# Moving bias, q and k loads, GpSimd's order and one weight split in a fused attention and two-MoE kernel

## The chip, the core and the metric

The kernel runs on one core of one Trainium2 chip. The metric is the device time of the whole launch in microseconds (us), lower is better. TensorE (PE) multiplies and transposes, VectorE (DVE), ScalarE (ACT) and GpSimd (POOL) work elementwise, and SyncE (SP) issues nearly all DMAs. Each engine runs its own instructions in order and waits on semaphores.

## What is computed

Attention with a learned relative bias, then two feed-forward layers. The reference, cut to what matters:

```python
# q, k, v: (4, 8, 576, 64); hidden = 32
scores = scale * np.matmul(q, k.transpose(0, 1, 3, 2))
rel = (pos[:, None] - pos[None, :])
x = (log1p(abs(rel)) / log1p(max(pos[:, None], 1)))[..., None]
bias = np.maximum(x @ w1 + b1, 0.0) @ w2          # (576, 576, 8)
scores = scores + bias.transpose(2, 0, 1)[None]
attn = softmax(scores)
o = attn @ v                                      # -> x: (2304, 512)
h = maximum(maximum(x @ m1, x @ m2), x @ m3)      # d_ff 768
x = h @ m_out
h = x @ m2_in                                     # d_ff 2048
g = where(h >= 1, h, where(h <= -1, 0, (h + 1)**2 / 4))
out = g @ m2_out
```

## The kernel before

Everything is float32. A product is made in three passes over a high part and a low part of each operand (`_hi` and `_lo`, rounded value and rest). The program has four stages: the bias, attention, the first feed-forward layer (C) and the second (D).

**Bias stage.** 36 steps `s` make 16 rows of the bias for all 8 heads each. Per step VectorE fills three quarters of the hidden tile (L830) and ScalarE one (`hidden_act`, L544), TensorE multiplies (L1027), ScalarE copies the result from PSUM into one of four staging buffers (`bias_copy`, L553), and SyncE stores it to `bias_scratch` in DRAM (`store_bias`, L362, 296 KB). The copy of step s may not start before the store of step s-4 has landed, which is the semaphore `bias_free[s % 4]`. The bias is then read back tile by tile: `first_bias(h, t, stored)` waits until the first `stored` stores have landed and loads tile t (128 rows, the last one 64) for head h of the pair, as one DMA (h = 0, L352, 288 KB) or two (h = 1, L354 and L355, 256 and 32 KB). All of this stands on SyncE's one queue in program order, between stores, together with `load_q` (four DMAs, L312 and L314) and `load_k` (five, L320 to L327) of the first pairs of heads.

**Attention.** 16 pairs of heads (`GROUPS`) with 5 row tiles each (`NT`) give 80 tiles. Work is laid out in slots `w` = 0 to 82: in slot w TensorE makes the scores of tile w (L941), turns the probabilities of tile w-3 (`turn_probs`, L954, and L968), turns q and k for a tile further on (`turn_rest`, L917) and does a piece of the product with v (L993). VectorE adds the bias and takes the row extreme (`add_bias`, L760), inverts the denominator of tile w-1 (L790), and copies half of the turned probabilities of tile w-3 (`copy_lower`, L774). ScalarE copies the other half (L589), copies turned q, k (`copy_turned`, L603 and L609) and takes the exponents (L577). GpSimd makes the high and low parts of turned q and k (`high_turned` L471, `low_turned` L480), normalises tile w-1 (`normalise`, L497), and prepares the denominator of tile w (`denominators`, L488). `high_turned(w)` waits, in every slot with w % 5 == 3, for the scores of tile w+1, since it overwrites what these read.

**Attention's end.** Weights of the layers come as units of 1024 columns: loaded into one of two buffers `raw`, split by ScalarE into the high part (`split_weights`, L639) and by VectorE (L823) or GpSimd (L516) into the low part. A load of unit u waits until unit u-2 is split. `W_SPLIT` is slot 75. Units 0 and 1 are split in slots 75 to 79; unit 2 only after the last output copy (L781) of attention, because its place in `w_all` overlaps attention tiles that are still in use. The slots 80 to 82 of TensorE already hold the first three products of layer C; the next ones (L1041) need unit 2.

## Time and profile before

| | us |
|---|---|
| median of 3 runs (1034.73 to 1037.45) | 1035.3 |
| the profiled execution | 1034.67 |
| its span | 1032.5 |
| TensorE busy in the span | 998.2 (97%) |
| VectorE / ScalarE / GpSimd busy | 506.6 / 493.5 / 294.8 |
| bias stage | 0 to 62 |
| attention | 62 to 329 |
| layers C and D | from 332 |

The profiled execution is 0.6 below the median and 2.2 above its own span. Since TensorE is busy nearly all the time from 77 us on, the columns to look at are the idle time before its instructions and what ended it; in the first 62 us TensorE, VectorE and ScalarE share the load, and the DMA engines are busy at 0.74 of the time.

### The profile page before, as it was taken

How to read it: one execution, taken by the hardware profiler on the slowest of the kernel's cores; microseconds unless marked ns; L12 is line 12 of the kernel's file. 1: busy time of each engine (PE TensorE's matmuls, PEld its weight loads, DVE VectorE, ACT ScalarE, POOL GpSimd, SP SyncE). 2: the span in 40 equal slices, each digit the busy share in tenths (PEclk: the TensorE clock that was granted, in tenths of full speed). 3: DMA queues.
4: the chain of work that ended last, by engine and by line, in shares of the span. 5: the costliest groups of instructions: out<-in, count | busy, mean ns of one | idle time of the engine just before them, and what ended most of it. 6: DMA issues, size and time to landing. Idle time of an engine off the chain costs nothing.

```text
span 1032.5 us, 20383 instructions
## 1 busy us (share of the span) xinstructions
PE 998.2 (97%) x7608; PEld 866.3 (84%) x7608; DVE 506.6 (49%) x1173; ACT 493.5 (48%) x1024; POOL 294.8 (29%) x506
## 2 busy tenths in 40 slices
PE   6779999999998999999999999999999999999998
PEld 4457666677666999999999999998989989899897
DVE  8867667666683231323131326754444444544543
ACT  7888777787793321212121325544343433433433
POOL 1048888888883720000000235700000000000000
PEclk9989999999999999999999999999999999999999
DMA  5872524425311410000000112300000000000000
GB/s 141 260 217 65 150 67 102 125 48 161 93 34 50 143 41 1 1 0 0 0 0 0 41 62 82 103 1 31 1 31 0 0 30 0 30 0 0 31 1 31
DMA packets 96042, 56.10 MB, mean 54 GB/s; under 512 B 64224, under 2 KB 81632, under 8 KB 95968
## 3 DMA queue, kind: packets, MB, share of 16 engines
q1 hardware_dynamic: 95872, 55.11, 19.0%
q8 instruction: 46, 0.75, 0.3%
q14 instruction: 28, 0.23, 0.1%
q10 hardware_dynamic: 96, 0.00, 0.0%
HBM read 39.46 MB, written 15.63 MB: 53 GB/s over the span
## 4 chain that ended last, share of the span: by engine, by line
PE 90%; DVE 5%; issue 2%; ACT 1%; POOL 1%; SPq 0%; DMA 0%; ACTq 0%; DVEq 0%
PE ps L1041 41%; PE ps L1100 19%; PE ps L1068 7%; PE ps L993 7%; PE ps L941 7%; PE ps L954 3%; DVE xT L830 2%; PE ps L1027 2%; PE ps L968 1%; DVE s_sb L760 1%; PE ps L917 1%; ACT probs L577 0%; POOL probs L497 0%; ACT xT L544 0%; DVE w_all L823 0%
## 5 line engine op out<-in xcount | busy, mean ns | idle before, releaser
L1041 PE MATMUL ps<-x_hi,w_all 128*128 128x384 f32 x1632 | 437.9, 336 | 3.0 <-DVE w_all L823 3.0
L1041 PEld LDWEIGHTS ps<-x_hi,w_all 128*128 128x128 f32 x1632 | 297.1, 188 | 8.9 <-issue 4.7
L1041 PE MATMUL ps<-x_lo,w_all 128*128 128x384 f32 x816 | 273.3, 335 | 0.0
L1100 PE MATMUL ps<-w_all,g_hi 128*128 128x512 f32 x576 | 179.8, 393 | 0.0
L1041 PEld LDWEIGHTS ps<-x_lo,w_all 128*128 128x128 f32 x816 | 153.2, 188 | 3.9
L516 POOL TENSOR_TENSOR w_all<-raw,w_all 128x256 fp32r<-128x256 f32 x100 | 77.6, 808 | 274.6 <-ACT w_all L639 274.6
L760 DVE CUSTOM_DVE_ANT_0 s_sb<-ps,bias_h 128x576 f32<-128x576 f32 (+1 forms) x160 | 114.5, 752 | 47.3 <-PE ps L941 40.4
L497 POOL TENSOR_SCALAR probs<-probs,row_inv 128x576 f32<-128x576 f32 (+1 forms) x160 | 121.9, 771 | 4.8 <-DVE row_inv L790 4.8
L1100 PEld LDWEIGHTS ps<-w_all,g_hi 128*128 128x128 f32 x576 | 106.4, 188 | 19.2 <-issue 1.2
L577 ACT ACTIVATE probs<-s_sb,row_min 128x576 f32<-128x576 f32 (+1 forms) x160 | 122.2, 769 | 0.0
L1100 PE MATMUL ps<-w_all,g_lo 128*128 128x512 f32 x288 | 113.9, 395 | 0.0
L701 ACT ACTIVATE ta<-ps 128x384 f32<-128x384 f32 x96 | 47.0, 490 | 115.5 <-PE ps L1041 114.9
L883 DVE TENSOR_SCALAR tb<-ta 128x384 f32<-128x384 f32 x96 | 38.0, 396 | 113.8 <-ACT ta L701 112.0
L891 DVE TENSOR_TENSOR g_lo<-tb,g_hi 128x384 fp32r<-128x384 f32 x96 | 56.6, 589 | 58.6 <-ACT g_hi L711 58.6
L850 DVE TENSOR_TENSOR tb<-ps,ta 128x384 f32<-128x384 f32 x36 | 20.0, 555 | 126.8 <-PE ps L1041 126.8
L711 ACT ACTIVATE g_hi<-tb 128x384 fp32r<-128x384 f32 x96 | 50.4, 524 | 63.8 <-DVE tb L889 63.8
L1068 PE MATMUL ps<-g_hi,w_all 128*128 128x384 f32 x288 | 78.8, 334 | 0.0
L993 PE MATMUL ps<-p_t,v_in 128*64 128x320 f32 (+1 forms) x512 | 76.0, 418 | 0.6 <-DVE xT L781 0.6
L589 ACT ACTIVATE p_t<-ps 128x512 f32<-128x512 f32 x80 | 47.7, 597 | 56.7 <-PE ps L954 55.2
L705 ACT ACTIVATE tb<-tb 128x384 f32<-128x384 f32 x96 | 50.4, 525 | 48.8 <-DVE tb L883 48.8
L677 ACT ACTIVATE g_hi<-tc 128x384 fp32r<-128x384 f32 x36 | 18.9, 524 | 112.5 <-DVE tc L857 112.5
L889 DVE TENSOR_TENSOR tb<-tb,tc 128x384 f32<-128x384 f32 x96 | 56.4, 588 | 32.2 <-ACT tb L705 31.8
(78 smaller groups left out, 1325.7 us busy)
## 6 DMA issues: line engine op xcount, KB each, us to landing
bias_scratch<-p_t SPq DMA_DIRECT2D x36, 296.0 KB, 3.8
raw<-in_moe_w_out SPq DMA_DIRECT2D x22, 256.0 KB, 3.0
bias_h<-bias_scratch SPq DMA_DIRECT2D x16, 288.0 KB, 4.2
raw<-in_moe_w SPq DMA_DIRECT2D x18, 256.0 KB, 3.1
out<-o_sb SPq DMA_DIRECT2D x18, 256.0 KB, 2.0
q_in<-in_q SPq DMA_DIRECT2D x32, 128.0 KB, 2.4
bias_h<-bias_scratch SPq DMA_DIRECT2D x16, 256.0 KB, 3.4
v_in<-in_v SPq DMA_DIRECT2D x32, 128.0 KB, 2.4
```

What stands on the lines that cost most here:

```text
L497: pool.tensor_scalar(pr, pr, row_inv[0:n, r, h:h + 1], 1.0, ALU.mult, ALU.mult).then_inc(p_norm, 1)
L516: last = pool.tensor_tensor(w_lo[:, at + c:at + c + PIECE], raw[:, u % 2, c:c + PIECE], w_hi[:, at + c:at + c + PIECE].bitcast(F32), ALU.s ...
L577: act.activation(probs[0:n, r, h * S:(h + 1) * S], s_sb[0:n, (2 * u + h) % 4, :], ACT.Exp, scale=-1.0, bias=row_min[0:n, r, h:h + 1], accu ...
L705: act.activation(tb[:, :], tb[:, :], ACT.Square, scale=0.5, bias=0.5).then_inc(d_sq, 1)
L760: dve.tensor_tensor_reduce(s_sb[0:n, (2 * u + h) % 4, :].rearrange("p (c x) -> p c x", c=2), ps[0:n, 2 * h:2 * h + 2, 0:HC], bias_h[0:n, h ...
L889: dve.tensor_tensor(tb[:, :], tb[:, :], tc[:, :], ALU.add).then_inc(d_g, 1)
L891: dve.tensor_tensor(g_lo[:, ft % 4, :], tb[:, :], g_hi[:, ft % 4, :].bitcast(F32), ALU.subtract).then_inc(d_g_ok, 1)
L941: ends = [pe.matmul(ps[:, 2 * h + c, 0:HC], a[HALVES[h], i % 2, 0, t * P:(t + 1) * P], b[HALVES[h], i % 2, 1, c * HC:(c + 1) * HC], start= ...
L993: last = pe.matmul(ps[h * HALF:(h + 1) * HALF, O_BANK_A, 0:cols.stop - cols.start], v_in[:, i % 2, h, kt, :], tqk[:, i % 2, 0, cols] if kt ...
L1041: last = pe.matmul(ps[:, bank, 0:BLK], w[:, at:at + P], x[:, kt, :], start=(kt == 0 and n == 0), stop=(kt == KT - 1 and n == 2))
L1068: last = pe.matmul(ps[:, Y_BANK + dt, 0:BLK], w[:, at:at + P], g[:, ft % 2, :], start=(opens and i == 0), stop=(closes and i == 2))
L1100: last = pe.matmul(ps[:, O_BANK + t, :], g[:, ft % 4, t * P:(t + 1) * P], w[:, wout_d(ft):wout_d(ft) + DM], start=(opens and i == 0), stop ...
```

## The change

There are five edits. In the diff the first `slot` is GpSimd's, the second ScalarE's. (1) SyncE loads tiles 1 (both heads) only after stores 33 and 34, and tiles 2 and 3 after the last store, instead of during the stage; tile 0 stays after stores 11 and 12. `load_v(0)` goes ahead of the tiles 4. (2) The q and k of the third pair, loaded after the stage before, are now loaded after store 22 (q) and store 26 (k). (3) In the first two slots ScalarE takes the exponents before it copies the turned q and k, and GpSimd normalises and prepares the denominator before it makes the high and low parts. (4) GpSimd has this second order also in every slot with w % 5 == 3. (5) `qk_hi` and `qk_lo` move behind the other tiles of attention in memory, so that unit 2's place is free after the last scores; its high part is made in slot 80 and its low part in slot 82, and unit 1's low part moves from slot 79 to slot 80.

```diff
             v_in = sb("v_in", [P, 2, 2, NT, D], c=att)
-            qk_hi = sb("qk_hi", [P, 2, 2, NT * P], F32R, c=att)
-            qk_lo = sb("qk_lo", [P, 2, 2, NT * P], F32R, c=att)
...
             row_inv = sb("row_inv", [P, RING, 2], c=att)
+            qk_hi = sb("qk_hi", [P, 2, 2, NT * P], F32R, c=att)
+            qk_lo = sb("qk_lo", [P, 2, 2, NT * P], F32R, c=att)
...
-                if i >= 2:
+                if i >= 3:
                     sp.wait_ge(lo_ok, NT * (i - 1))
...
-                if s > 4 and (s - 4) % 8 == 7:
-                    first_bias(0, (s - 4) // 8, s - 3)
-                if s > 4 and (s - 4) % 8 == 0:
-                    first_bias(1, (s - 4) // 8 - 1, s - 4)
-            first_bias(1, T - 1, NSUP - 4)
-            load_qk(2)
+                if s == 22:
+                    sp.wait_ge(lo_ok, NT)
+                    load_q(2)
+                if s == 26:
+                    load_k(2)
+                if s in (11, 12):
+                    first_bias(s - 11, 0, s - 3)
+                if s in (NSUP - 3, NSUP - 2):
+                    first_bias(s - NSUP + 3, 1, 2 * P // SUP)
+            for t in range(2, T):
+                for h in range(2):
+                    first_bias(h, t, (t + 1) * P // SUP)
+            sp.wait_ge(staged_zero, 1)
+            load_v(0)
             for h in range(2):
                 first_bias(h, T, NSUP)
-            sp.wait_ge(staged_zero, 1)
-            load_v(0)
...
             def slot(w):
-                high_turned(w)
-                if w < 2:
-                    low_turned(w)
+                late = w < 2 or w % NT == 3
+                if not late:
+                    high_turned(w)
                 if w:
                     normalise(w - 1)
                 if w < NU:
                     denominators(w)
-                if w >= 2:
-                    low_turned(w)
+                if late:
+                    high_turned(w)
+                low_turned(w)
...
             def slot(w):
-                copy_turned(w)
+                if w >= 2:
+                    copy_turned(w)
                 if w < NU:
                     exponent(w, 0)
                     exponent(w, 1)
+                if w < 2:
+                    copy_turned(w)
...
-                if w in (W_SPLIT, W_SPLIT + 2):
+                if w in (W_SPLIT, W_SPLIT + 2, W_SPLIT + 5):
                     split_weights((w - W_SPLIT) // 2)
             act.wait_ge(o_ok, PAIRS)
-            split_weights(2)
...
-                if w in (W_SPLIT + 2, W_SPLIT + 4):
-                    low_weights((w - W_SPLIT - 2) // 2)
+                if w - W_SPLIT in (2, 5, 7):
+                    low_weights((2, 5, 7).index(w - W_SPLIT))
             output(GROUPS - 1, 0)
             output(GROUPS - 1, 1)
-            low_weights(2)
```

SyncE's queue from the tenth to last store of the bias stage on, before (after the k load of the second pair; `x7` are stores 21 to 27, then 29 to 35):

```order
34 L362 DMA bias_scratch<-p_t 16x8x592 x7
35 L352 DMA bias_h<-bias_scratch 128x576
36 L362 DMA bias_scratch<-p_t 16x8x592
37 L354 DMA bias_h<-bias_scratch 128x512
38 L355 DMA bias_h<-bias_scratch 128x64
39 L362 DMA bias_scratch<-p_t 16x8x592 x7
40 L352 DMA bias_h<-bias_scratch 128x576
41 L354 DMA bias_h<-bias_scratch 128x512
42 L355 DMA bias_h<-bias_scratch 128x64
43 L312 DMA q_in<-in_q 128x4x64
```

The same place now (`x4` are stores 23 to 26, `x7` are 27 to 33; four q DMAs stand ahead of the first row):

```order
34 L362 DMA bias_scratch<-p_t 16x8x592 x4
35 L320 DMA k_in<-in_k 128x4x64
36 L322 DMA k_in<-in_k 64x64
37 L325 DMA k_in<-in_k 64x4x64
38 L326 DMA k_in<-in_k 64x4x64
39 L327 DMA k_in<-in_k 64x64
40 L362 DMA bias_scratch<-p_t 16x8x592 x7
41 L352 DMA bias_h<-bias_scratch 128x576
42 L362 DMA bias_scratch<-p_t 16x8x592
43 L354 DMA bias_h<-bias_scratch 128x512
44 L355 DMA bias_h<-bias_scratch 128x64
45 L362 DMA bias_scratch<-p_t 16x8x592
```

The k load now stands between store 26 and store 27, and no bias load stands between store 12 and store 33.

GpSimd in its fourth slot (w = 3), before: high part, two normalisations, denominator, low part:

```order
27 L471 TENSOR_SCALAR qk_hi<-tqk 128x2x128
28 L497 TENSOR_SCALAR probs<-probs,row_inv 128x576 x2
29 L488 TENSOR_SCALAR row_den<-row_sum 128x2
30 L480 TENSOR_TENSOR qk_lo<-tqk,qk_hi 128x2x128
31 L471 TENSOR_SCALAR qk_hi<-tqk 128x2x128
```

The same slot now (the functions stand six lines further down in the file):

```order
27 L503 TENSOR_SCALAR probs<-probs,row_inv 128x576 x2
28 L494 TENSOR_SCALAR row_den<-row_sum 128x2
29 L477 TENSOR_SCALAR qk_hi<-tqk 128x2x128
30 L486 TENSOR_TENSOR qk_lo<-tqk,qk_hi 128x2x128
31 L477 TENSOR_SCALAR qk_hi<-tqk 128x2x128
```

The high part, which waits for TensorE, moved behind the denominator. The same happens in slots 8, 13 and so on up to 68.

VectorE at attention's end (from slot 79's copy of turned probabilities), before; L823 is a low part of a weight unit, L781 an output copy:

```order
573 L774 COPY p_t<-ps 128x8x64 [waits py_ps]
574 L823 TENSOR_TENSOR w_all<-raw,w_all 128x1024 [waits w_ok,w_hi_ok]
575 L781 COPY xT<-ps 128x320 [waits o_ps]
576 L790 RECIPROCAL row_inv<-row_den 128x2 [waits p_norm,den_ok]
577 L774 COPY p_t<-ps 128x8x64 [waits py_ps] x2
578 L781 COPY xT<-ps 128x256 [waits o_ps]
579 L781 COPY xT<-ps 128x320 [waits o_ps]
580 L823 TENSOR_TENSOR w_all<-raw,w_all 128x1024 [waits w_ok,w_hi_ok]
```

And now (L832 is the low part, L790 the output copy, L783 the copy of turned probabilities, L799 the inverse):

```order
573 L783 COPY p_t<-ps 128x8x64 [waits py_ps]
574 L790 COPY xT<-ps 128x320 [waits o_ps]
575 L799 RECIPROCAL row_inv<-row_den 128x2 [waits p_norm,den_ok]
576 L783 COPY p_t<-ps 128x8x64 [waits py_ps]
577 L832 TENSOR_TENSOR w_all<-raw,w_all 128x1024 [waits w_ok,w_hi_ok]
578 L783 COPY p_t<-ps 128x8x64 [waits py_ps]
579 L832 TENSOR_TENSOR w_all<-raw,w_all 128x1024 [waits w_ok,w_hi_ok]
580 L790 COPY xT<-ps 128x256 [waits o_ps]
```

The output copy is no longer behind unit 1's low part, and unit 2's low part stands ahead of both last output copies instead of behind them.

## Rows read from the trace of the kernel before

**Rows 1.** Windows: us, then each engine's busy time, PE clock, DMA share, GB/s.
```profile
0.00:62.20 62.20, 46.62 (x894) 26.97 (x894) 49.65 (x116) 51.27 (x78) 3.43 (x16) 1.00 0.74 211
62.20:77.40 15.20, 11.09 (x106) 9.02 (x106) 8.82 (x26) 11.67 (x28) 11.00 (x22) 0.78 0.71 185
77.40:300.00 222.60, 217.06 (x2644) 154.38 (x2643) 157.19 (x440) 177.07 (x430) 189.56 (x352) 1.00 0.38 96
...
332.00:1032.50 700.50, 695.97 (x3708) 656.52 (x3706) 273.66 (x553) 236.43 (x451) 77.37 (x100) 1.00 0.08 25
```

**Rows 2.** Waits, 24 to 62.2 us: who waited for whom: total, times, longest.
```profile
ACT p_t L553 <- DMA bias_scratch<-p_t: 5.5, 5, 2.8
```

**Rows 3.** Timeline of ScalarE: start, us, ..., [idle before <- what ended it].
```profile
46.29 0.76 ACT L553 ACTIVATE p_t<-ps,nconst 128x592 f32<-128x592 f32 x1 [0.38 <-DMA bias_scratch<-p_t]
...
48.43 0.75 ACT L553 ACTIVATE p_t<-ps,nconst 128x592 f32<-128x592 f32 x1 [0.73 <-DMA bias_scratch<-p_t]
...
49.75 0.74 ACT L553 ACTIVATE p_t<-ps,nconst 128x592 f32<-128x592 f32 x1
...
56.99 0.75 ACT L553 ACTIVATE p_t<-ps,nconst 128x592 f32<-128x592 f32 x1 [0.42 <-DMA bias_scratch<-p_t]
```

**Rows 4.** Timeline of SyncE's queue around the second pair's k load.
```profile
31.75 0.60 SPq L320 DMA_DIRECT2D k_in<-in_k  x1
...
35.40 1.24 SPq L362 DMA_DIRECT2D bias_scratch<-p_t  x2
```

**Rows 5.** DMA issues, last us to landing: the stores issued at 24.9 and 35.4.
```profile
bias_scratch<-p_t SPq DMA_DIRECT2D x1, 296.0 KB, 3.1
...
bias_scratch<-p_t SPq DMA_DIRECT2D x1, 296.0 KB, 4.0
```

**Rows 6.** The same view: store 33 (issued at 60.7), tile 3's last piece (64.6).
```profile
bias_scratch<-p_t SPq DMA_DIRECT2D x1, 296.0 KB, 4.2
...
bias_h<-bias_scratch SPq DMA_DIRECT2D x1, 32.0 KB, 4.0
```

**Rows 7.** Timeline at attention's start: scores of tiles 3, 4; bias add of tile 3.
```profile
69.37 0.40 PE L941 MATMUL ps<-qk_hi 64*128 64x288 f32 x2 [1.55 <-DVE row_min L760]
...
71.90 0.75 DVE L760 CUSTOM_DVE_ANT_0 s_sb<-ps,bias_h 128x576 f32<-128x576 f32 x1
...
72.81 0.61 PE L941 MATMUL ps<-qk_hi 64*128 64x288 f32 x2
```

**Rows 8.** Timeline of GpSimd, VectorE, TensorE in a group in the middle.
```profile
153.86 0.40 POOL L471 TENSOR_SCALAR qk_hi<-tqk 128x256 fp32r<-128x256 f32 x1 [1.56 <-PE ps L941]
...
156.02 0.17 DVE L790 RECIPROCAL row_inv<-row_den 128x2 f32<-128x2 f32 x1 [0.86 <-POOL row_den L488]
156.10 0.67 DVE L774 COPY p_t<-ps 128x512 f32<-128x512 f32 x1
...
156.42 0.29 PE L941 MATMUL ps<-qk_lo,qk_hi 64*128 64x288 f32 x2
156.55 0.29 PE L941 MATMUL ps<-qk_hi,qk_lo 64*128 64x288 f32 x2
156.92 0.28 PE L954 MATMUL ps<-ident,probs 64*128 64x64 f32 x2
```

**Rows 9.** Waits, 84 to 300 us.
```profile
PEld ps L954 <- issue: 3.6, 13, 0.3
```

**Rows 10.** Timeline of attention's end.
```profile
312.84 1.21 DVE L823 TENSOR_TENSOR w_all<-raw,w_all 128x1024 fp32r<-128x1024 f32 x1
...
314.60 1.08 PE L993 MATMUL ps<-p_t,v_in 128*64 128x256 f32 x8 [0.56 <-DVE xT L781]
...
329.21 1.06 ACT L639 ACTIVATE w_all<-raw 128x1024 fp32r<-128x1024 f32 x1 [5.57 <-DVE xT L781]
330.18 0.47 ACT L666 ACTIVATE ta<-ps 128x384 f32<-128x384 f32 x1
...
331.63 0.41 PE L1041 MATMUL ps<-x_hi,w_all 128*128 128x384 f32 x1 [2.99 <-DVE w_all L823]
```

## The prediction

> **What bounds the kernel now.** I read the busy times by stretch first [rows 1]. From 332 us on TensorE is busy for 695.97 of 700.5 us, so nothing before it matters there except when it begins. From 77.4 to 300 it is busy for 217.06 of 222.6: about 5.5 us idle, which an order of the other engines can give back. The first 62.2 us are another thing: TensorE 46.6, VectorE 49.7, ScalarE 51.3, DMA share 0.74. There ScalarE's copies wait for stores, 5.5 us in 5 waits [rows 2]. The stretch from 62.2 to 77.4 is the ramp of attention: TensorE has 4.1 of 15.2 us idle and a mean granted clock of 0.78. The end of attention has one large gap, 2.99 us [rows 10]. The change touches all four places, and since TensorE sets the end from 77 us on, what each place gives to or takes from TensorE adds up.
>
> **Bias stage.** A copy of step s needs the store of step s-4. Of the 5.5 us, three waits of 0.38, 0.73 and 0.42 (1.5 us) come after 46 us [rows 3]. The other two (5.5 - 1.5 = 4.0, one of them 2.8) come earlier, from tile 0's loads and the second pair's k load, and both loads stay where they are: cost unchanged. The waits at 46.29 and 48.43 are those for stores 20 and 21, which shared the DMA engines with tile 1's loads. Those loads leave, so 0.38 + 0.73 = 1.1 us go, and copy 26 starts at 48.65 instead of 49.75 and ends at 49.4.
>
> What comes in their place is the k load after store 26. The five DMAs keep SyncE for 35.40 - 31.75 = 3.65 us [rows 4], so from 49.4 + 0.6 on it is occupied until about 53.3, and store 27 goes out only then. A store that follows such a load landed after 3.1 us (behind a q load) or after 4.0 (behind the k load) [rows 5]: store 27 lands at 56.4 to 57.7. Copy 31 needs it. Without any wait it would start at 56.99 - 0.42 - 1.1 = 55.5 [rows 3], so it waits for 0.9 to 2.2 us and starts at 56.4 to 57.7, against 56.99 before. From the copy of step 31 on ScalarE works through without a wait. The stage ends 0.6 us earlier to 0.7 later; I take **0.0**, the middle. The new q load after store 22 delays store 23 in the same way by some 2.4 us, but copy 27 falls at about 50 and store 23 should have landed at 50.1 to 51; I put this into the range (up to +1.0), not the sum.
>
> A rule speaks against this exchange. The q and k rows are 64 floats, 256 bytes, whereas a bias row has 2304. The trace shows no penalty of its own: the store behind four q DMAs took 3.1 us, as short as the shortest. The Trainium skill (DMA: Bandwidth & Descriptors, Why small descriptors are slow (HBM only)) gives a fixed per-packet cost that makes a 256-byte one about 27% dearer. By that rule the q and k loads would cost the engines an extra quarter of their bytes' time, which would make the stage's term the upper end instead of zero.
>
> **First tiles.** Tiles 1 to 3 now come after store 33. Store 33 went out at 60.7 and landed 4.2 later, at 64.9; tile 3's last piece went out at 64.6 and landed at 68.6 [rows 6]. Between the two landings lie two stores and two loads, 3.7 us, 0.93 each. Now two stores and six loads lie behind store 33: 8 x 0.93 = 7.4 us, tile 3's last piece lands at 72.3; with loads a little dearer than stores, at 73. The bias of tile 3 is added after it, 0.75 us a head [rows 7] (the scores of tile 3 started at 69.37 after waiting 1.55 us for tile 2's add), and the scores of tile 4 start after that, at 73.1 to 73.8, instead of 72.81. Tile 2's last piece lands two loads earlier, at 70.4 to 71, so tile 3's scores start at 71.2 to 71.8 instead of 69.37, and everything TensorE does behind them until tile 4 (3.4 us before) comes later by that, if it does not find time: 73.8 to 75.2. ScalarE's and GpSimd's new order takes a wait away here, since normalising tile 0 no longer stands behind the low parts of slot 1; it is hidden, because the loads are last. About half of the lag falls into the time at half clock, and counts half at full clock. I take **+1.0** (0 to +2.4).
>
> **GpSimd's fourth slot.** Before, GpSimd waits 1.56 us for the scores of tile w+1 with the normalisation and the denominator behind it. So VectorE's inverse waits 0.86 us for the denominator, the copy behind it ends at 156.10 + 0.67 = 156.77, and TensorE's transposes, which need that copy, issue at 156.92 [rows 8]. The two score instructions ahead of them stand 0.13 apart; the transposes follow after 0.37. Without the wait they would follow after 0.13 as well: 0.24 us. The view of waits counts 13 of these between 84 and 300, 3.6 us, 0.28 each [rows 9]. After the change the denominator is ready before the wait, the inverse and the copy come 0.8 us earlier, and the wait for the scores falls into time that GpSimd has. Since TensorE is bound everywhere behind, the 0.24 pass on: 13 x 0.24 = 3.1. I take **-3.0**; the bounds are 0 (another wait takes its place) and -3.6. The high parts that now come later are those of a group two further on, so nobody waits for them.
>
> **Attention's end.** Two pieces. Output copy L781 was late since it stood behind unit 1's low part (1.21 us), and TensorE waited 0.56 for it [rows 10]: this goes, -0.5. The low part now stands behind it; its first user is TensorE's third product, two slots further on. And the gap before 331.63: TensorE is idle since 328.64. After the change unit 2 is ready long before; what is late next is ScalarE's copy of the first product (L666, 0.47 us), which still waits for the last output copy, that is until 329.21, and before the next product may overwrite the bank. It ends at 329.68, and TensorE starts at about 329.7 instead of 331.63: -1.9. Next behind is unit 3's low part, on GpSimd: it starts a good microsecond earlier too and is wanted two products (4.2 us) after the restart; the slack is small and may cost 0.3. Together **-2.4** (-1.8 to -2.6).
>
> **The sum.** 0.0 + 1.0 - 3.0 - 2.4 = -4.4 us. Against the profiled execution's own time, 1034.67, that is 1030.3; it stood 0.6 below the median of 1035.3, so I predict **1030.9** for the median.
>
> **Rivals.** (a) The fourth slot gives nothing: GpSimd was never last, or the wait returns a tile later, since TensorE's handover to the fourth tile of each group already waits for VectorE. Against it: each link from GpSimd to TensorE has its row. Then -1.4, 1033.9. (b) The late loads cost the ramp 2 us more than I say, or the lower clock lasts longer. In the stretch from 62.2 to 77.4 the granted clock is first the full 2.4 GHz and then 1.2, 0.78 in the mean [rows 1], after TensorE had waited in turns for the bias adds; its first score instruction took 0.61 us at 72.81 instead of 0.40 [rows 7]. If it stays low for three slots more, at 0.7 us each, this costs 2.1. Then -2.3, 1033.0. The Trainium skill (TensorE: Matmul & The Clock Gate, Part 1) says that activity releases the throttle and that the point of the turn is free-running, so that it varies between runs; that would let both outcomes occur with the same kernel. (c) The stage gains fully: store 27 lands early enough and ScalarE runs through, -1.5 more, 1029.4. (d) Slower than before: the six loads behind store 33 queue so long that attention's start is late by more than the other terms give. The other terms give 5.4, of which my +1.0 for a landing at 73 is taken; so it decides from a landing at 77.4, that is from (77.4 - 64.9 - 1.9) / 6 = 1.8 us for each of the six loads. With 2.5 us each it would be 81.8 and the time 1035.3 + 4.4 = 1039.7. The two loads in [rows 6] took about 1 each.
>
> **How the numbers follow.** My forecast 0.60, (a) 0.13, (b) 0.14, (c) 0.10, (d) 0.03. A measurement of this kernel tells about 0.3%, 3.1 us, from no change. The forecast's own range, -6 to -2.8, lies nearly all beyond that, (c) does, (b) and (a) do not: faster 0.70, same 0.27, slower 0.03. The range reaches from (c) to between (a) and (b): 1028.8 to 1033.9.
>
> **What the profile after would show.** Right: no wait of the transposes once per group, and no inverse waiting 0.86; the gap at the end of attention 1.0 or less; no gap before the first product with v in slot 80. ScalarE's copy of step 31 waiting for a store by about 1 to 2 us, and none at steps 24 and 25. Scores of tiles 2 and 3 waiting for bias adds that wait for a DMA. Wrong would be: the group's period unchanged at its steady rate, the gap at the end ended by GpSimd's low part, or tile 4's scores starting later than 75.5.

## The result, and the profile after

| | us |
|---|---|
| kernel after, median of 8 runs (1029.5 to 1032.63) | 1031.64 |
| kernel before, median of 8 runs of the same set (1033.86 to 1037.45) | 1035.33 |
| ratio after / before | 0.9958, 95% interval 0.9946 to 0.9971 |
| profiled execution after, its span | 1032.09, 1029.9 |
| profiled execution before, its span | 1034.67, 1032.5 |

The ratio is 0.42% or 4.35 us (3.0 to 5.6), the two medians lie 3.7 apart and the two profiled executions 2.6.

Windows of the kernel after, with the columns of [rows 1]; the second begins where TensorE starts the scores of tile 0:

```profile
0.00:64.70 64.70, 47.19 (x882) 27.02 (x882) 49.64 (x116) 50.50 (x77) 3.43 (x16) 0.95 0.70 194
64.70:77.40 12.70, 8.99 (x89) 7.17 (x81) 6.02 (x18) 9.25 (x21) 7.93 (x16) 0.77 0.86 255
77.40:300.00 222.60, 217.40 (x2680) 157.21 (x2682) 155.91 (x447) 180.07 (x438) 193.81 (x358) 1.00 0.39 96
300.00:332.00 32.00, 29.96 (x282) 21.94 (x279) 18.56 (x42) 18.83 (x43) 14.23 (x20) 1.00 0.19 56
332.00:1029.90 697.90, 693.39 (x3693) 653.82 (x3691) 272.68 (x551) 234.69 (x448) 75.46 (x98) 1.00 0.07 24
```

Attention starts at 64.7 instead of 61.2, and the granted clock of the bias stage is no longer full (0.95). The starts of the scores of four tiles, read from TensorE's timeline, show where the two profiles differ:

| | tile 0 | tile 3 | tile 8 | tile 73 | products of C go on |
|---|---|---|---|---|---|
| before | 61.16 | 69.37 | 85.60 | 291.22 | 331.63 |
| after | 64.74 | 73.59 | 89.26 | 291.20 | 329.02 |
| difference | +3.6 | +4.2 | +3.7 | 0.0 | -2.6 |

Up to tile 8 the new kernel loses 3.7 us, 3.6 of them before the first scores. The 13 groups from tile 8 to tile 73 win back 3.7, and attention's end wins 2.6.

**The stage.** Waits of ScalarE from 24 to 66 us (total, times, longest), and then its copies of steps 25, 27, 31 and 35 in the timeline, which answer to [rows 2, 3]:

```profile
ACT p_t L560 <- DMA bias_scratch<-p_t: 8.0, 8, 2.0
ACT p_t L560 <- PE ps L1035: 1.1, 1, 1.1
```
```profile
49.02 0.75 ACT L560 ACTIVATE p_t<-ps,nconst 128x592 f32<-128x592 f32 x1 [0.71 <-DMA bias_scratch<-p_t]
...
52.25 0.75 ACT L560 ACTIVATE p_t<-ps,nconst 128x592 f32<-128x592 f32 x1 [0.49 <-DMA bias_scratch<-p_t]
...
59.58 0.75 ACT L560 ACTIVATE p_t<-ps,nconst 128x592 f32<-128x592 f32 x1 [1.81 <-DMA bias_scratch<-p_t]
...
64.86 0.76 ACT L560 ACTIVATE p_t<-ps,nconst 128x592 f32<-128x592 f32 x1 [1.10 <-PE ps L1035]
```

SyncE's queue before store 27, against [rows 4]:

```profile
51.71 0.79 SPq L320 DMA_DIRECT2D k_in<-in_k  x1
...
54.92 1.46 SPq L327 DMA_DIRECT2D k_in<-in_k  x1
56.42 7.25 SPq L362 DMA_DIRECT2D bias_scratch<-p_t  x7
```

The k load holds SyncE from 51.71 to 56.42. Store 27 is then 3.1 us on its way, as the DMA view says of the stretch from 56.4 to 56.9:

```profile
bias_scratch<-p_t SPq DMA_DIRECT2D x1, 296.0 KB, 3.1
```

56.42 + 3.1 is the 59.5 at which the copy of step 31 starts, after the longest wait of the late stage. Where the 3.6 us come from, wait by wait: step 31 1.81 instead of 0.42, step 27 0.49 instead of none, step 35 1.10 instead of none, step 24 none instead of 0.38: together 2.6. The remaining 1.0 is there at the copy of step 20 already (41.87 instead of 40.77), ahead of anything that the change moves; in the nine kernels that are the same up to there, this copy starts between 40.16 and 41.87. So the moved loads themselves account for 1.5 of the 3.6. Of the 2.6, the 1.10 of step 35 is a wait for a product that TensorE made at half clock: from 62.2 us on the granted clock stood at 1.2 GHz for 3.4 us, of which this window of the stage's end shows a part:

```profile
62.20:64.70 2.50, 2.36 (x36) 1.24 (x28) 0.00 (x0) 1.56 (x3) 0.00 (x0) 0.50 0.77 223
```

**The first tiles.** Landing of store 33 (issued in the stretch from 63.1 to 63.5) and of tile 3's last piece (69.6 to 69.9), as in [rows 6]:

```profile
bias_scratch<-p_t SPq DMA_DIRECT2D x1, 296.0 KB, 4.5
...
bias_h<-bias_scratch SPq DMA_DIRECT2D x1, 32.0 KB, 4.5
```

Bias adds of tile 2's second head and the scores of tiles 3 and 4, as in [rows 7]:

```profile
72.09 0.76 DVE L769 CUSTOM_DVE_ANT_0 s_sb<-ps,bias_h 128x576 f32<-128x576 f32 x1 [1.21 <-DMA bias_h<-bias_scratch]
...
73.59 0.61 PE L949 MATMUL ps<-qk_hi 64*128 64x288 f32 x2 [0.88 <-DVE row_min L769]
...
77.15 0.61 PE L949 MATMUL ps<-qk_hi 64*128 64x288 f32 x2
```

VectorE now waits for a load, which it never did before: from tile 0's scores to tile 3's it takes 8.85 us instead of 8.21.

**The steady group.** TensorE, GpSimd and VectorE in the slot that answers to [rows 8]:

```profile
159.07 0.30 PE L949 MATMUL ps<-qk_hi,qk_lo 64*128 64x288 f32 x2
159.20 0.66 PE L962 MATMUL ps<-ident,probs 64*128 64x64 f32 x16
```
```profile
155.69 0.19 POOL L494 TENSOR_SCALAR row_den<-row_sum 128x2 f32<-128x2 f32 x1
156.37 0.40 POOL L477 TENSOR_SCALAR qk_hi<-tqk 128x256 fp32r<-128x256 f32 x1 [0.48 <-PE ps L949]
```
```profile
157.60 0.15 DVE L799 RECIPROCAL row_inv<-row_den 128x2 f32<-128x2 f32 x1
```

The transposes (L962) follow the last score instruction after 0.13 us instead of 0.37; the inverse waits for nothing. In the waits from 84 to 300 us the row of [rows 9] is gone, and so is VectorE's wait for the denominator (24.6 us in 60 times before). GpSimd's wait for the scores was 20.5 us in 13 times and is now:

```profile
POOL qk_hi L477 <- PE ps L949: 5.8, 13, 0.5
```

**The end.** The output copy, the copy of the first product and TensorE's restart, against [rows 10]:

```profile
327.86 0.49 DVE L790 COPY xT<-ps 128x320 f32<-128x320 f32 x1 [4.73 <-PE ps L1001]
```
```profile
328.38 0.49 ACT L675 ACTIVATE ta<-ps 128x384 f32<-128x384 f32 x1 [5.57 <-DVE xT L790]
```
```profile
329.02 0.41 PE L1049 MATMUL ps<-x_hi,w_all 128*128 128x384 f32 x1 [1.21 <-ACT ta L675]
```

The gap is 1.21 us instead of 2.99 and ends with ScalarE's copy of the first product, which waits for the last output copy. The gap of 0.56 before a product with v is gone: the product that answers to it starts at 313.77 without a wait.

### The profile page after: what moved, and what is told of

Read it like the earlier page. It is cut to its first block, busy times and chain, and to the rows that moved or that the text cites. A ratio compares the mean times of both kernels' runs of the same rounds, so it can differ in the third digit from the quotient of the medians.

```text
span 1029.9 us, 20383 instructions
## 1 busy us (share of the span) xinstructions
PE 996.9 (97%) x7608; PEld 867.2 (84%) x7608; DVE 502.8 (49%) x1173; ACT 493.3 (48%) x1024; POOL 294.9 (29%) x506
## 4 chain that ended last, share of the span: by engine, by line
PE 73%; DVE 1%; issue 0%; POOL 0%; ACT 0%; ACTq 0%; DVEq 0%
PE ps L1049 42%; PE ps L1108 20%; PE ps L1076 7%; PE ps L1001 2%; PE ps L949 1%; PE ps L962 1%; DVE s_sb L769 0%; POOL probs L503 0%; PE ps L976 0%; PE ps L925 0%; DVE p_t L783 0%; DVE row_min L769 0%; DVE x_lo L824 0%; ACT o_sb L729 0%; DVE xT L790 0%
## 5 line engine op out<-in xcount | busy, mean ns | idle before, releaser
L769 DVE CUSTOM_DVE_ANT_0 s_sb<-ps,bias_h 128x576 f32<-128x576 f32 (+1 forms) x160 | 114.8, 753 | 78.3 <-PE ps L949 62.2
```

Source lines behind the costliest of these rows:

```text
L769: dve.tensor_tensor_reduce(s_sb[0:n, (2 * u + h) % 4, :].rearrange("p (c x) -> p c x", c=2), ps[0:n, 2 * h:2 * h + 2, 0:HC], bias_h[0:n, h ...
```

## The experiments

Twelve kernels ran in four sets, each set beside the kernel before (medians 1035.62, 1037.14, 1036.01 and 1035.45). Times of different sets are compared by their ratios; a difference of two ratios is good to some 1.8 us.

| kernel | median | ratio (95%) | tile 0 | tile 0 to 3 | tile 3 to 8 | half clock, 55 to 86 us |
|---|---|---|---|---|---|---|
| before | | | 61.16 | 8.21 | 16.23 | 6.8 |
| after | 1031.64 | 0.9958 (0.9946 to 0.9971) | 64.74 | 8.85 | 15.67 | 10.2 |
| f1_pool | 1030.39 | 0.9953 (0.9940 to 0.9966) | 61.60 | 8.21 | 15.12 | 3.4 |
| f2_unit2 | 1032.46 | 0.9967 (0.9952 to 0.9981) | 62.16 | 8.20 | 16.35 | 6.8 |
| f3_no_sp | 1029.52 | 0.9936 (0.9922 to 0.9949) | 61.41 | 8.19 | 17.95 | 10.2 |
| f4_sp_only | 1040.16 | 1.0043 (1.0031 to 1.0055) | 63.00 | 10.36 | 16.35 | 10.2 |
| g1_qk_late | 1033.65 | 0.9969 (0.9957 to 0.9981) | 59.88 | 10.60 | 20.39 | 17.0 |
| g2_qk_inside | 1033.73 | 0.9968 (0.9956 to 0.9980) | 65.03 | 8.18 | 17.79 | 10.2 |
| g3_spread2 | 1029.67 | 0.9928 (0.9914 to 0.9942) | 61.07 | 10.48 | 15.56 | 10.2 |
| g4_spread1 | 1027.89 | 0.9911 (0.9898 to 0.9925) | 59.32 | 8.20 | 17.95 | 10.2 |
| h1_no_first2 | 1026.58 | 0.9905 (0.9888 to 0.9921) | 60.02 | 8.20 | 15.52 | 3.4 |
| h2_filler | 1026.01 | 0.9905 (0.9890 to 0.9920) | 57.72 | 9.00 | 15.70 | 0 |
| h3_tile2_late | 1026.88 | 0.9910 (0.9893 to 0.9926) | 58.51 | 8.95 | 16.73 | 13.7 |
| h4_filler_early | 1026.44 | 0.9909 (0.9893 to 0.9926) | 59.79 | 8.32 | 16.40 | 3.4 |

The columns of tiles are starts of scores in TensorE's timeline of the profiled execution; the last is how long the granted clock stood at 1.2 GHz there.

### One edit at a time

**f1_pool**: the kernel before with edit (4) alone.

```diff
-                high_turned(w)
+                late = w % NT == 3
+                if not late:
+                    high_turned(w)
...
+                if late:
+                    high_turned(w)
```

> The kernel before with GpSimd's new order in the slots with w % 5 == 3 alone. Theory A (each edit counts by its own rows): the wait of the transposes goes in 13 to 14 groups at 0.24 to 0.28 us, so -3.1 to -3.9 us against before, and a group takes 15.5 us instead of 15.8; the gap before 331 us stays at 3.0. Theory B (the wait only goes together with the other edits, or comes back a tile later): 0 to -1 us.

Measured: 0.9953, 4.9 us less (3.5 to 6.2). Tile 8 to tile 73 take 201.91 us instead of 205.62: 3.71. GpSimd's wait, in the waits from 84 to 297 us, is nearly the row of the kernel after:

```profile
POOL qk_hi L471 <- PE ps L945: 5.6, 12, 0.5
```

So the edit does alone what it does in the whole. Rival (a) is out.

**f2_unit2**: the kernel before with edit (5) alone, the move in memory and unit 2's split.

```diff
-                if w in (W_SPLIT, W_SPLIT + 2):
+                if w in (W_SPLIT, W_SPLIT + 2, W_SPLIT + 5):
...
-            split_weights(2)
...
-                if w in (W_SPLIT + 2, W_SPLIT + 4):
-                    low_weights((w - W_SPLIT - 2) // 2)
+                if w - W_SPLIT in (2, 5, 7):
+                    low_weights((2, 5, 7).index(w - W_SPLIT))
...
-            low_weights(2)
```

> The kernel before with qk_hi and qk_lo moved in memory and unit 2's split inside attention alone. Theory A: -1.9 for the gap before layer C, which falls from 3.0 to 1.1, and -0.5 for the wait in slot 80, together -2.4 to -2.6 us; a group stays at 15.8 us. Theory B (a low part on GpSimd or a later load eats it): -1 us or less.

Measured: 0.9967, 3.4 us less (2.0 to 5.0). From tile 73 to the restart TensorE takes 38.10 us instead of 40.41, 2.3 less, with the gap again 1.21 us. The 13 groups do not change (205.67), and GpSimd's wait, from 84 to 300 us, stays:

```profile
POOL qk_hi L471 <- PE ps L939: 20.6, 13, 1.7
```

**f3_no_sp**: the kernel after with SyncE's order of before, that is edits (3), (4) and (5) without (1) and (2).

```diff
-                if s == 22:
-                    sp.wait_ge(lo_ok, NT)
-                    load_q(2)
-                if s == 26:
-                    load_k(2)
...
+                if s > 4 and (s - 4) % 8 == 7:
+                    first_bias(0, (s - 4) // 8, s - 3)
+                if s > 4 and (s - 4) % 8 == 0:
+                    first_bias(1, (s - 4) // 8 - 1, s - 4)
+            first_bias(1, T - 1, NSUP - 4)
+            load_qk(2)
```

> The changed kernel with SyncE's loads in the order of the kernel before (the first-slot order, the fourth-slot order and unit 2 as changed). Theory A, in which SyncE's new order costs what the profile after shows at the first tiles (some 3 us late by slot 8): -6 to -7 us against before, 2 to 3 us faster than the changed kernel. Theory B, in which that lateness was the chance of one execution (slower DMA landings, clock at half around 42 and 62 us) and SyncE's new order is worth nothing or a little: about -3.7 to -4.5, as the changed kernel.

Measured: 0.9936, 6.6 us less than before (5.3 to 8.1), and 2.3 less than the kernel after by the two ratios, which is little more than the 1.8 that such a difference is good to.

**f4_sp_only**: the kernel before with edits (1) and (2) alone, the reverse of the diff above.

> The kernel before with SyncE's new order of loads alone (tiles 1 to 3 of the bias after store 33, q and k of the third pair after stores 22 and 26). Theory A: +2 to +3.5 us, with ScalarE's copy of step 31 waiting for store 27 by 1 to 2 us and the bias adds of tiles 1 to 3 waiting for their loads. Theory B: within 1 us of before. My prediction's terms for it were 0.0 and +1.0.

Measured: 1.0043, **4.5 us slower** than before (3.2 to 5.7). VectorE's waits from 59 to 76 us name the cost in the ramp; the kernel before has no such row:

```profile
DVE s_sb L766 <- DMA bias_h<-bias_scratch: 4.6, 3, 1.9
```

Tile 0 to tile 3 take 10.36 us, 2.15 more than before, and the stage ends 1.8 later. It is not the clock: with the same mean granted clock of 0.997, one run of this kernel took 1038.6 us and three of the kernel before in this set 1034.0 to 1035.4. So SyncE's new order costs, and edits (4) and (5) carry the whole gain. The three effects measured alone, -4.9, -3.4 and +4.5, make -3.8, and the kernel after has -4.35 (-5.6 to -3.0): the sum fits.

### What in SyncE's order costs

**g1_qk_late**: the kernel after, but the third pair's q and k loads come after the stage again. The bias loads stay late.

```diff
-                if s == 22:
-                    sp.wait_ge(lo_ok, NT)
-                    load_q(2)
-                if s == 26:
-                    load_k(2)
...
                 for h in range(2):
                     first_bias(h, t, (t + 1) * P // SUP)
+            sp.wait_ge(lo_ok, NT)
+            load_q(2)
+            load_k(2)
```

> The changed kernel, but with q and k of the third pair loaded after the bias stage again (between the loads of tiles 3 and of v); the bias loads stay late. Theory K (the q and k loads inside the stage, which hold SyncE back from its stores, are what the new load order costs in the stage): the stage ends 1.5 to 2.5 us earlier than in the changed kernel, no wait of ScalarE at copies 27 and 31, and the time falls by 1.5 to 2.5 us, to about -6 us against before. Theory L (the late bias loads are the whole cost): the stage ends as in the changed kernel and the time is within 0.7 us of it.

Measured: 0.9969, so 3.4 us worse than f3_no_sp and no better than the kernel after (0.9958), against theory K. Its stage does come as theory K has it: no wait at copy 27, 0.32 at copy 31, and tile 0 at 59.88 instead of 64.74 in the kernel after. But the ramp, tile 0 to tile 8, takes 30.99 us instead of 24.52 there and 26.14 in f3_no_sp. VectorE's waits from 59 to 76 us, and its first bias add of tile 4:

```profile
DVE s_sb L767 <- DMA bias_h<-bias_scratch: 2.9, 2, 1.5
...
78.36 0.75 DVE L767 CUSTOM_DVE_ANT_0 s_sb<-ps,bias_h 64x576 f32<-64x576 f32 x1 [3.80 <-DMA bias_h<-bias_scratch]
```

The longest wait is for the load of tile 4. It stands behind the late bias loads, the nine DMAs of q and k and the four of v, and goes out only at 74.57; TensorE waits 3.40 us for this add. So this kernel moves a cost as well as removing one, and part of its ramp is a longer half clock (17.0 us). It does not price the late bias loads alone.

**g2_qk_inside**: f3_no_sp with edit (2) alone: the bias loads inside the stage as before, the q and k loads inside too.

```diff
+                if s == 22:
+                    sp.wait_ge(lo_ok, NT)
+                    load_q(2)
+                if s == 26:
+                    load_k(2)
...
-            load_qk(2)
```

> The kernel with SyncE's old order (f3_no_sp, -6.6 us against before) with only the q and k loads of the third pair moved inside the stage, bias loads as before. Theory K: +1.5 to +3 us against f3_no_sp, so -3.5 to -5 us against before, with more waits of ScalarE for stores after copy 26. Theory L: within 0.7 us of f3_no_sp, -6 to -7 against before.

Measured: 0.9968, 3.3 us worse than f3_no_sp, and all of it is in the stage: tile 0 at 65.03 instead of 61.41, tile 0 to tile 3 unchanged. ScalarE's copies of steps 31 and 32:

```profile
59.48 0.75 ACT L558 ACTIVATE p_t<-ps,nconst 128x592 f32<-128x592 f32 x1 [2.22 <-DMA bias_scratch<-p_t]
...
61.91 0.75 ACT L558 ACTIVATE p_t<-ps,nconst 128x592 f32<-128x592 f32 x1 [0.94 <-DMA bias_scratch<-p_t]
```

Is it the bytes, or SyncE held for five DMAs in a row? **g3_spread2**: the kernel after with the same nine DMAs in the same part of the stage, but one behind each of stores 20 to 28.

```diff
-                if s == 22:
+                if s == 20:
                     sp.wait_ge(lo_ok, NT)
-                    load_q(2)
-                if s == 26:
-                    load_k(2)
+                if 20 <= s < 24:
+                    load_q(2, (s - 20,))
+                if 24 <= s < 29:
+                    load_k(2, (s - 24,))
```

> The changed kernel with the nine DMAs of the third pair's q and k put one by one behind stores 20 to 28 instead of four behind 22 and five behind 26; the bytes and the bias loads are the same. Theory K1 (what costs is SyncE being occupied for 3.7 us in a row, so that store 27 goes out late): copy 31's wait falls from 1.8 to under 0.5 us and the time by 1 to 2 us against the changed kernel. Theory K2 (what costs is the traffic on the DMA engines): the waits spread over more copies, and the time stays within 0.7 us.

Measured: 0.9928, 3.1 us better than the kernel after. SyncE's queue, in which a store now waits behind one DMA instead of five:

```profile
48.26 1.35 SPq L330 DMA_DIRECT2D k_in<-in_k  x1
49.66 0.58 SPq L365 DMA_DIRECT2D bias_scratch<-p_t  x1
50.29 0.60 SPq L330 DMA_DIRECT2D k_in<-in_k  x1
50.93 0.60 SPq L365 DMA_DIRECT2D bias_scratch<-p_t  x1
```

Its copy of step 31 waits for nothing, and ScalarE's waits for stores from 24 to 66 us are 3.9 us instead of 8.0. The bytes are the same; what cost was the row of DMAs.

The four experiments are best compared from the start of step 20's copy to that of step 33's, which leaves out what differed before the moved loads. From ScalarE's timelines:

| between these copies | kernels | us |
|---|---|---|
| bias loads, as before | before, f1_pool, f2_unit2, f3_no_sp | 19.13, 19.01, 19.23, 19.65 |
| neither bias loads nor q and k | g1_qk_late | 18.37 |
| q and k in two rows | after, f4_sp_only | 20.51, 20.87 |
| q and k in two rows, and bias loads | g2_qk_inside | 22.31 |
| q and k spread | g3_spread2 | 18.22 |

Taking the bias loads out gave about 1 us, putting q and k in as two rows cost 2 to 3, and spread out they cost nothing that shows.

**g4_spread1**: f3_no_sp with the same done to the second pair's loads, which the change did not touch: q behind stores 5 to 8, k behind stores 13 to 17.

```diff
-                if s == 8:
-                    load_q(1)
-                if s == 14:
-                    load_k(1)
+                if 5 <= s < 9:
+                    load_q(1, (s - 5,))
+                if 13 <= s < 18:
+                    load_k(1, (s - 13,))
```

> SyncE's old order (f3_no_sp) with the q and k loads of the second pair put one by one behind stores 5 to 8 and 13 to 17, instead of together behind 8 and 14. Theory K1: the waits at copies 19 and 20, 2.8 us together in f3_no_sp, fall to under 1 us, the stage ends about 1.5 to 2 us earlier, -8 us against before; that would be the fastest version. Theory K2: within 0.7 us of f3_no_sp.

Measured: 0.9911, 2.6 us better than f3_no_sp and 9.2 better than before. Tile 0 starts at 59.32. The waits of steps 19 and 20, 2.8 us in f3_no_sp, are gone.

### The first two slots and the clock

**h1_no_first2**: g4_spread1 without edit (3).

```diff
-                late = w < 2 or w % NT == 3
+                late = w % NT == 3
...
-                low_turned(w)
+                if w >= 2:
+                    low_turned(w)
...
-                if w >= 2:
-                    copy_turned(w)
+                copy_turned(w)
...
```

> The kernel with the new order in GpSimd's fourth slots, the new end of attention and the second pair's q and k loads spread one by one behind stores, but with ScalarE and GpSimd ordered in the first two slots as in the kernel before. Theory: the order in the first two slots is worth nothing, because the scores of tile 0 to those of tile 3 take 8.2 us with it (59.32 to 67.52) and without it (61.16 to 69.37, kernel before): the time is within 1 us of the 1027.9 of the same kernel with the new order, ratio to before 0.990 to 0.992, and the scores of tile 0 to tile 3 again take 8.2 us. Rival: the new order takes a wait off GpSimd that only its absence shows: 1 to 2 us slower, ratio 0.993.

Measured: 0.9905 against 0.9911, no difference that this can tell, and tile 0 to tile 3 take 8.20 us in both. No worth of edit (3) shows. It may even bring a small wait: where it is combined with q and k loaded after the stage (f3_no_sp, g4_spread1, h2_filler, h3_tile2_late), TensorE waits 0.3 to 1.3 us for the third pair's k, and in the kernels without it never. No run was made for this.

In f3_no_sp and g4_spread1 the half clock in the ramp lasts 10.2 us, in h1_no_first2 and f1_pool 3.4. **h2_filler** asks whether it follows from TensorE's idle time: g4_spread1 with six added matmuls in each of slots 0 to 3, into a bank unused then. It computes more, and the output is unchanged.

```diff
                 turn_rest(w)
+                if w < 4:
+                    for n in range(6):
+                        pe.matmul(ps[:, O_BANK_A, 0:HC], qk_hi[HALVES[0], 0, 0, 0:P],
+                                  qk_hi[HALVES[0], 0, 1, 0:HC], start=True, stop=True)
```

> The kernel with the spread loads plus six matmuls of 128x256 in each of slots 0 to 3 into a bank that nobody uses then; they add work and change no output. Theory: the half-clock stretch at 69 to 79 us (10.2 us there) follows from TensorE's idle time in the ramp; filled, the granted clock stays at 2.4 GHz, the scores of tile 4 to those of tile 8 take 11 us instead of 14.7, and the time falls by 2 to 3 us to about 1025.5, ratio 0.989. Rival 1: the stretch comes whatever TensorE does and only its place varies: half clock of 3.4 to 10.2 us again, the time up by the filler that finds no idle time, 0 to 1.5 us. Rival 2: more activity brings it earlier, into slots 0 to 3, and it costs 1 to 3 us more.

Windows of g4_spread1, h1_no_first2 and h2_filler, one each, around the half-clock stretch, with the columns of [rows 1]:

```profile
69.00:79.30 10.30, 9.05 (x73) 6.83 (x71) 6.25 (x18) 6.59 (x15) 9.15 (x18) 0.51 0.48 111
```
```profile
69.80:73.20 3.40, 3.30 (x31) 2.81 (x33) 2.45 (x7) 2.17 (x5) 3.15 (x7) 0.50 0.54 131
```
```profile
66.70:79.80 13.10, 11.01 (x148) 8.76 (x148) 8.45 (x25) 9.98 (x25) 12.36 (x24) 1.00 0.49 114
```

With the filler the clock stays at 2.4 GHz: the mean granted clock of its four timed runs is 0.999 to 1.0, against 0.994 to 0.998 in the five of g4_spread1. Tile 3 to tile 8 take 15.70 us instead of 17.95. But 0.8 of it is paid between tile 0 and tile 3 (9.00 instead of 8.20), and the ratio, 0.9905, can't be told from the 0.9911 of g4_spread1 or the 0.9905 of h1_no_first2, both without any filler. The theory holds for the clock and not for the size of its gain. The filler comes after the scores of tile 0, so it can't be why these start at 57.72 here and at 59.32 in g4_spread1: in the four kernels with this same stage (g4_spread1, h1_no_first2 and both fillers) they start between 57.72 and 60.02. A difference of 2 us in the stage between single profiles is chance unless a wait accounts for it.

**h4_filler_early**: h1_no_first2 with the same filler ahead of `turn_rest`, where TensorE waits for ScalarE's copy.

```diff
                     turn_probs(tile_of(w))
+                if w < 4:
+                    for n in range(6):
+                        pe.matmul(ps[:, O_BANK_A, 0:HC], qk_hi[HALVES[0], 0, 0, 0:P],
+                                  qk_hi[HALVES[0], 0, 1, 0:HC], start=True, stop=True)
                 turn_rest(w)
```

> The kernel with GpSimd's new order in the fourth slots only, the new end of attention and the second pair's q and k loads spread, with the order of the first two slots as in the kernel before, plus the six added matmuls in slots 0 to 3, now ahead of the turning of q and k, where TensorE waits 1.0 us a slot for ScalarE's copy. They add work and change no output. Six take 6 x 0.13 = 0.8 us. Theory: here they find idle time, the scores of tile 0 to tile 3 take 8.2 to 8.5 us instead of the 9.0 with them behind the turning, and the granted clock stays full in every run (0.999 or 1.0 in the mean, against 0.996 to 0.997 without them): 0.5 to 1.5 us below the 1026.6 of the same kernel without them, about 1025.5, ratio 0.989 to 0.990. Rival 1: the half clock comes again, since what fills the gap is too early or too short: mean clock 0.996 or less and the time unchanged. Rival 2: the full clock is kept but the added work is on the path: scores of tile 0 to tile 3 9.0 us or more, time within 0.5 of 1026.6 or above.

Measured: 0.9909, mean clock 0.998 to 1.0 in its four runs. Tile 0 to tile 3 take 8.32 us, so the work does find idle time there. Then a new wait appears, in TensorE's groups from 57 to 80 us:

```profile
L959 PE MATMUL ps<-ident,probs 64*128 64x64 f32 x56 | 2.9, 250 | 1.3 <-POOL probs L500 1.3
```

The transposes wait 1.3 us for GpSimd, and tile 3 to tile 4 take 4.33 us instead of 3.46. No gain of either filler was shown.

**h3_tile2_late**: g4_spread1 with only tile 2's bias loads taken out of the stage.

```diff
-                if s > 4 and (s - 4) % 8 == 7:
+                if s in (11, 19):
                     first_bias(0, (s - 4) // 8, s - 3)
-                if s > 4 and (s - 4) % 8 == 0:
+                if s in (12, 20):
                     first_bias(1, (s - 4) // 8 - 1, s - 4)
+                if s in (33, 34):
+                    first_bias(s - 33, 2, 24)
```

> The kernel with the spread loads, and tile 2's bias loads taken from behind stores 27 and 28 to behind stores 33 and 34, tile 1's and 3's staying. Theory: one tile's loads out of the stage give 0.5 to 0.8 us there (both tiles' gave 1.6), and the queue behind store 33 has only three more DMAs, all landed by the time tile 2's bias is added: the scores of tile 0 start at 58.5 to 58.8, tile 3's 8.2 to 9 us later, the time 0 to 0.8 lower than 1027.9. Rival: as with all late loads, the scores of tile 3 wait for the bias: 9.5 us or more from tile 0's scores, and 1 to 2 us slower.

Measured: 0.9910, the same. Tile 0 starts at 58.51, 0.8 earlier, which is inside the spread of the four kernels above and shows nothing; tile 0 to tile 3 take 0.75 more. VectorE waits for no load in this ramp, but its half clock began early, at 62.7, and which of the two the 0.75 belongs to stays open.

The five kernels from g4_spread1 on, 0.9905 to 0.9911, can't be told apart; each is 9 to 10 us faster than before, and their intervals lie below that of the kernel after.

## Why the prediction was right, and one of its terms wrong

The time (1031.64, predicted 1030.9) and the sign came out, out of two gains that were sized a little low or well and one loss that was sized too low. The closeness of the sum is in part luck: two errors of opposite sign stand against each other.

- **Fourth slot, -3.0 predicted.** Measured -3.7 in the profile (201.94 instead of 205.62 us) and again in f1_pool. Every link that the prediction named is in the rows: the denominator before the wait, the inverse without a wait, transposes 0.13 behind the scores. What it mis-sized is the amount per group: it took the 0.24 between two starts, while the period of a group fell by 3.68 / 13 = 0.28, the figure that the wait had in [rows 9]. The bound of -3.6 was the better value.
- **Attention's end, -2.4 predicted.** Measured -2.6 in the profile and -2.3 in f2_unit2. What is late next is ScalarE's copy of the first product, as said, at 328.38. TensorE starts 0.15 behind its end. Unit 3's low part costs nothing.
- **Bias stage, 0.0 predicted. This is the term that failed.** Copy 31 was to start at 56.4 to 57.7 and started at 59.58, and at 58.85 in f4_sp_only, which has the same order in SyncE's queue. What it mis-sized is how long the k load holds SyncE: 3.65 us was taken from the second pair's load, and the third pair's held it for 4.71 (51.71 to 56.42), 4.79 in f4_sp_only and 4.45 in g2_qk_inside. (The recorded working also loses 0.35: 50.0 + 3.65 is 53.65, not 53.3.) Store 27 then landed after the 3.1 us assumed. Second, the q load, left out of the sum, makes copy 27 wait 0.49 (1.00 in f4_sp_only). Third, the wait of step 25 did not go as reckoned, 0.71 against 0.73 in [rows 3]; but it is 0.22 in f4_sp_only and nothing in g3_spread2, while the five kernels with tile 1's loads in place have 0.73 to 1.17, so on the whole this gain was there. By the table under g3_spread2 the moved loads cost the stage 1.4 to 1.7 us over the kernel before, above the upper end of +1.0. The rest of the 3.6 us was chance: 1.0 before step 20, and 1.10 for a product at half clock, which f4_sp_only does not have.
- **The rule on small rows** was set against the trace with "upper end" for the stage. The end did come, and higher, but not by that rule: spread over nine places, the same 256-byte rows cost nothing that shows (18.22 us with them, 18.37 without, in the table). What the Trainium skill (DMA: Bandwidth & Descriptors, Why small descriptors are slow (HBM only)) says of bytes on the engines decided nothing here; what decided is how long the issuing queue is held ahead of a store. The 3.1 us of the store behind the q load was not quite the shortest landing, as the prediction has it: a store issued between 49.2 and 50 us landed after 3.0.
- **First tiles, +1.0 predicted.** In the kernel after, tile 0 to tile 8 take 24.52 us against 24.44. Alone it is dearer: the kernels with late bias loads take 2.2 to 2.4 more from tile 0 to tile 3 (10.36, 10.60, 10.48 against 8.2), and the kernel after only 0.64. Its loads had a start, since the first of them was issued at 63.82, 0.9 before the scores of tile 0, whereas in f4_sp_only, g1_qk_late and g3_spread2 it was issued 0.1 behind them (at 63.08, 59.99 and 61.16). So the late end of the stage may hide a part of the late loads; that fits the four kernels, but no run was made for it alone, and the start came from the chance wait of step 35. There is a rival: in those three kernels 4.1 to 5.7 us of tile 0 to tile 3 ran at half clock, in the kernel after 2.0. In h3_tile2_late 4.7 us of it went with 0.75 more, so it can be a part, but not all, of the 2.2 to 2.4. The queue itself was reckoned well: from the landing of store 33 (about 67.6) to that of tile 3's last piece (74.1) it took 6.5 us, against 7.4 predicted.
- **Rivals.** (a) fell by f1_pool. (b) was half there: the ramp took over 2 us more wherever the stage was not late too, loads and half clock together. (c) fell: the stage gained nothing. (d), slower than before, did not come for the whole, but f4_sp_only shows that for the SyncE edits taken alone it is the true case, at +4.5 us, and not by the queue of loads that it has in mind: it is the sum of a held queue and waits for loads of up to 1.9 us.
- **Signs.** One of the three signs of being wrong came: tile 4's scores were not to start after 75.5, and they started at 77.15, since tile 0's started 3.6 late. Step 25 was to have no wait and has one, and the gap at the end is 1.21, not 1.0 or less. The others came as said.

As a whole, SyncE's order was put at +1.0 and cost 4.5 alone (3.2 to 5.7), 2.3 beside the other edits. The other terms, -5.4 predicted, were -6.3 in the profile and -6.6 in f3_no_sp. The sum is nearer the truth than its terms.

Open: why the third pair's k load holds SyncE 1 us longer than the second pair's, why the wait of step 25 stayed in the kernel after and not in f4_sp_only, and why step 20's copy starts up to 1.7 us apart in kernels that are the same up to there.

## What to carry to other kernels

Count what a moved load does to the queue that issues it before counting its bytes: several small DMAs in a row delay the next store by their issue time, and if that store frees a buffer, the engine behind it waits for what the other buffers don't cover (here the queue was held for 4.7 us and the copy waited 1.8). Spreading them one behind each store gave 3.1 and 2.6 us in two places, each good to 1.8. Look also at what stands behind the moved loads in their new place: in g1_qk_late that was tile 4's bias, and it cost 3.4 us. When one diff holds several edits, time each alone: here two edits carried the whole gain, one showed nothing, and the two of SyncE took some back. Without these three and with the loads spread, h1_no_first2 has 0.9905 where the kernel after has 0.9958.

## What the runs showed of the chip

The granted clock of TensorE in attention's ramp differs between executions of the same program, and in the kernel before the time goes with it. In its 32 timed executions in the first three sets, the four with a mean granted clock of 0.991 took 1037.6 to 1039.1 us and the four with 0.997 took 1034.0 to 1035.4. The 0.006 between them are 0.006 x 1033 / 0.5 = 12.4 us more at 1.2 GHz, and the means are 3.3 us apart (1038.1 and 1034.8). In the five runs of f1_pool and the six of f2_unit2 (0.994 to 1.0) no such relation shows, and a mean clock does not say where the half clock lay. In seven of the 14 profiled executions (after, f1_pool to f4_sp_only, g1_qk_late, g3_spread2) 3.4 us of it lay between 35 and 46 us, in the bias stage, where it made no difference that shows: from copy 20 to copy 33, f1_pool took 19.01 us with it and the kernel before 19.13 without. Attention's end can have it too: in f4_sp_only TensorE comes back from the 2.99 us gap at attention's end with a first product of 0.66 us instead of the 0.41 in [rows 10], and the window from 332 to 338 us shows 0.79:

```profile
335.90 0.66 PE L1047 MATMUL ps<-x_hi,w_all 128*128 128x384 f32 x1 [2.99 <-DVE w_all L829]
```

The kernel before and f1_pool have the same gap and the full clock behind it, so it is not the rule either. The Trainium skill (TensorE: Matmul & The Clock Gate, Part 1) has activity release the throttle and lets the point of the turn vary between runs. The traces agree with both: the same program with 0.991 and 0.997, and 0.998 to 1.0 in all eight runs with a filler. That a full clock is worth little when the work that buys it is on the path is what the two filler runs add.
